# The second block's rows turned by VectorE, and the turn of x between the two low parts, in a fused attention and expert kernel

## The reference

```python
# attention: state = gamma * state + k v^T ; y = scale * q state
# layer 2:   h = relu(x @ w_in); x = (h * sigmoid(conv(h))) @ w_out
def _moe2_ref(x, w_gate, w_local, w1, w2):
    ...
            fresh_e = int(np.argmax(logits[b, s]))
            if s == 0 or local_gate[b, s] < 0.5:
                e = fresh_e
            else:
                e = prev_e if prev_e >= 0 else fresh_e
            ...
            h = np.maximum(x[b, s] @ w1[e], 0.0)
            out[b, s] = p[e] * (h @ w2[e])
```

## Time and profile before

| | us |
|---|---|
| median of 3 runs | 425.1 |
| lowest and highest run | 423.46, 425.39 |
| the profiled execution | 423.02 |
| its span, first to last instruction | 420.5 |
| TensorE busy in the span | 406.0 |
| VectorE busy | 238.8 |
| ScalarE busy | 211.0 |
| GpSimd busy | 100.7 |

### The profile page before, as it was taken

How to read it: one execution, slowest core, us unless ns; L and a number is a source line. 1 busy time by engine, 2 the same in 40 slices (tenths; PEclk the granted TensorE clock), 3 DMA queues, 4 the chain that set the end, 5 groups by cost and what they waited for, 6 DMA issues and landing times.

```text
span 420.5 us, 7363 instructions
## 1 busy us (share of the span) xinstructions
PE 406.0 (97%) x2637; PEld 333.1 (79%) x2638; DVE 238.8 (57%) x309; ACT 211.0 (50%) x293; POOL 100.7 (24%) x104
## 2 busy tenths in 40 slices
PE   7999999999999999999999999999989999999992
PEld 3888799887889987778787778787667878777782
DVE  4888749982004977686277622118773274663761
ACT  2344678670115764561557432338763284755661
POOL 3354782000000000027621412221122222031220
PEclk9999999999999999999999999999999999999998
DMA  8999900000520009555474932225786367493720
GB/s 292 408 410 416 383 1 2 0 2 0 200 101 0 2 0 389 211 202 163 130 287 149 400 129 94 75 100 203 299 311 244 100 235 307 128 399 127 258 87 4
DMA packets 28442, 76.16 MB, mean 181 GB/s; under 512 B 4927, under 2 KB 14399, under 8 KB 24064
## 3 DMA queue, kind: packets, MB, share of 16 engines
q1 hardware_dynamic: 25216, 67.26, 42.1%
q0 software_dynamic: 2912, 8.13, 5.8%
q10 hardware_dynamic: 288, 0.41, 0.3%
HBM read 62.68 MB, written 14.42 MB: 183 GB/s over the span
## 4 chain that ended last, share of the span: by engine, by line
PE 84%; ACT 7%; issue 3%; ACTq 1%; DMA 1%; DVE 1%; POOL 0%; DVEq 0%; POOLq 0%
PE ps L1039 23%; PE ps L1043 22%; PE ps L1040 22%; ACT wx L616 4%; PE ps L1312 4%; PE ps L1071 3%; PE ps L1092 3%; PE ps L1089 2%; PE ps L1055 1%; PE ps L1138 1%; DMA kv<-qkv 1%; ACT os L681 1%; DVE xF L957 1%; ACT hs L664 1%; ACT hT L674 1%
## 5 line engine op out<-in xcount | busy, mean ns | idle before, releaser
L970 DVE TENSOR_TENSOR hT<-ps,hT 128x512 fp32r<-128x512 f32 x34 | 23.5, 692 | 83.5 <-ACT hT L674 83.5
L951 DVE TENSOR_TENSOR wx<-raw_w,wx 128x1024 fp32r<-128x1024 f32 x56 | 65.1, 1220 | 2.8 <-ACT wx L616 2.8
L1039 PE MATMUL ps<-wx,hT 128*128 128x512 f32 x136 | 55.7, 409 | 0.3
L616 ACT CAST wx<-raw_w 128x1024 fp32r<-128x1024 f32 x56 | 55.0, 1046 | 0.0
L1043 PE MATMUL ps<-wx,hT 128*128 128x512 f32 x136 | 54.8, 403 | 0.0
L1043 PE MATMUL ps<-wx,xT 128*128 128x512 f32 x136 | 54.5, 401 | 0.0
L1039 PE MATMUL ps<-wx,xT 128*128 128x512 f32 x136 | 53.5, 393 | 0.0
L1040 PE MATMUL ps<-wx,hT 128*128 128x512 f32 x136 | 53.3, 392 | 0.0
L1040 PE MATMUL ps<-wx,xT 128*128 128x512 f32 x136 | 53.2, 391 | 0.0
L494 POOL DMA_INDIRECT out<-os,snow x16 | 18.8, 1176 | 104.9 <-ACT os L681 104.9
L1039 PE MATMUL ps<-x,win 128*128 128x384 f32 x128 | 43.2, 337 | 0.0
(11 more groups left out here) (165 smaller groups left out, 726.4 us busy)
## 6 DMA issues: line engine op xcount, KB each, us to landing
raw_w<-w_exp SPq DMA_DIRECT2D x28, 1024.0 KB, 7.1
qk<-qkv SPq DMA_DIRECT2D x7, 768.0 KB, 9.5
raw_first<-w_exp SPq DMA_DIRECT2D x4, 1024.0 KB, 7.7
x_block<-xg SPq DMA_DIRECT2D x16, 256.0 KB, 2.0
xq<-x_block SPq DMA_DIRECT2D x64, 64.0 KB
kv<-qkv SPq DMA_DIRECT2D x4, 768.0 KB, 11.2
x_rows<-x2n SPq DMA_DIRECT2D x11, 256.0 KB, 2.8
kv<-qkv SPq DMA_DIRECT2D x7, 384.0 KB, 10.0
```

Source lines behind the costliest of these rows:

```text
L616: nc.scalar.copy(wx[:, slot, 0, c], raw).then_inc(wx_hi[w], 1)
L951: nc.vector.tensor_tensor(wx[:, slot, 1, c], raw, wx[:, slot, 0, c].bitcast(F32), ALU.subtract).then_inc(w2_lo_dve if w else w1_lo_dve, 1)
L970: nc.vector.tensor_tensor(lo, psHT[:, 512 * a:512 * a + 512], hi.bitcast(F32), ALU.subtract).then_inc(hT_done, 1)
L1039: mm(o, lh, rl, start=first, stop=False)
```

## The change

- Block 1's rows are no longer turned by TensorE. SP's `step(0)` stores `xg` once both are there, `gathered` 32 and `x_first` 2 (the last x2 tile, over whose place `xq` lies, has been read by TensorE), and loads the quarters; VectorE turns them and ScalarE and VectorE take the high and low parts from `xF`, after both halves of block 0's h.
- SP issues both halves of `raw_w2` of expert 1 ahead of the last x2 half store, and `raw_w1` of expert 2 behind `step(0)`.
- VectorE's `turn_x(g+1)` goes between `h_lo(g,0)` and `h_lo(g,1)` in every block from 1 on.
- In an expert's first block ScalarE does relu(g,0) ahead of the evacuation, and h_hi(g,0) ahead of the last weight piece.
- In TensorE's first layer of block 0 the parts come in another order: the last rows go one part sooner, and the first half is complete after five parts instead of six.

```diff
@@ SP
                 if n == 0:
                     sp.wait_ge(gathered, 16)
-                    raw(1, 1, raw_w2, raw_w2_in, (0,))
+                    raw(1, 1, raw_w2, raw_w2_in)
             sp.wait_ge(x2_done, TT + 1)
-            sp.wait_ge(gathered, 32)
-            raw(1, 1, raw_w2, raw_w2_in, (1,))
-            raw(0, 2, raw_w1[0], raw_w1_in[0])
...
             def step(g):
                 sp.wait_ge(gathered, 16 * g + 32)
                 sp.wait_ge(x_turned, 16 * g + 32)
                 sp.dma_start(x_block, xg[:]).then_inc(x_stored, 16)
-                sp.wait_ge(x_stored, 16 * g)
+                sp.wait_ge(x_stored, 16 * g + 16)
                 for q in range(NQ):
                     sp.dma_start(xq[TR * q:TR * q + TR],
                                  x_block[:, P * q:P * q + P].rearrange("(b j) n -> j b n", j=TR)
                                  ).then_inc(quartered, 16)
+
+            sp.wait_ge(x_first, 2)
+            step(0)
+            raw(0, 2, raw_w1[0], raw_w1_in[0])
@@ GpSimd
-                pool.wait_ge(x_stored, 16 * g)
+                pool.wait_ge(x_stored, 16 * g + 16)
                 gather(g + 2)
...
             pool.wait_ge(tables, 1)
-            pool.wait_ge(gathered, 32)
-            pool.wait_ge(xg_free, 3)
+            pool.wait_ge(x_stored, 16)
             gather(2)
@@ ScalarE
             def first_step(g, e, slot):
+                relu(g, 0)
                 evac_before(g, o_done)
-                relu(g, 0)
+                h_hi(g, 0)
                 if e is not None:
                     weights_hi(0, e, slot, (3,))
-                h_hi(g, 0)
                 relu(g, 1)
                 h_hi(g, 1)
                 act.wait_ge(x_turned, 16 * g + 48)
-                x_hi(g + 1, xF[:].rearrange("p k t -> p (k t)"))
+                x_hi()
...
             relu(0, 1)
-            act.wait_ge(xg_free, 3)
-            x_hi(1, psXT)
             h_hi(0, 1)
+            act.wait_ge(x_turned, 48)
+            x_hi()
             weights_hi(0, 1, 1, (2, 3))
@@ VectorE
-            dve.sem_inc(x_turned, 48)
+            dve.sem_inc(x_turned, 32)
...
             def step(g):
                 h_lo(g, 0)
+                turn_x(g + 1)
                 h_lo(g, 1)
-                turn_x(g + 1, 64 * g)
-                x_lo(g + 1, xF[:].rearrange("p k t -> p (k t)"))
+                x_lo(g + 1)
...
             def first_step(g, e, slot):
                 h_lo(g, 0)
+                turn_x(g + 1)
                 if e is not None:
                     weights_lo(0, e, slot, (3,))
                 h_lo(g, 1)
-                turn_x(g + 1, 64 * g)
-                x_lo(g + 1, xF[:].rearrange("p k t -> p (k t)"))
+                x_lo(g + 1)
...
             h_lo(0, 0)
-            x_lo(1, psXT)
             h_lo(0, 1)
+            turn_x(1)
+            x_lo(1)
             weights_lo(0, 1, 1, range(4))
@@ TensorE
-                for k, a in ((0, 0), (0, 1), (1, 0), (1, 1), (2, 0), (3, 0), (2, 1), (3, 1)):
-                    if (k, a) == (1, 0):
+                for k, a in ((0, 0), (0, 1), (1, 0), (2, 0), (3, 0), (1, 1), (2, 1), (3, 1)):
+                    if (k, a) == (0, 1):
                         last_rows(TT - 1, TT + 1, (2, 3))
...
-                    if (k, a) == (2, 1):
+                    if (k, a) == (1, 1):
                         turn_h(0, 0)
...
             first_w1()
-            turn_x(gathered, 32)
             pe.wait_ge(o_done, 1)
```

More of the change, by code:

```diff
@@ L304, in build @@
         psEnd, psRow, psSlot, psInv = bank(6), bank(3), bank(7), bank(2)
-        psP1, psHT, psXT, psO = bank(0, 2), bank(2, 2), bank(4), bank(5)
+        psP1, psHT, psO = bank(0, 2), bank(2, 2), bank(5)
         def column_half(a, n):
@@ L386, in _, with step @@
                     sp.wait_ge(gathered, 16)
-                    raw(1, 1, raw_w2, raw_w2_in, (0,))
+                    raw(1, 1, raw_w2, raw_w2_in)
             sp.wait_ge(x2_done, TT + 1)
-            sp.wait_ge(gathered, 32)
-            raw(1, 1, raw_w2, raw_w2_in, (1,))
+            def step(g):
+                sp.wait_ge(gathered, 16 * g + 32)
+                sp.wait_ge(x_turned, 16 * g + 32)
+                sp.dma_start(x_block, xg[:]).then_inc(x_stored, 16)
+                sp.wait_ge(x_stored, 16 * g + 16)
+                for q in range(NQ):
+                    sp.dma_start(xq[TR * q:TR * q + TR],
+                                 x_block[:, P * q:P * q + P].rearrange("(b j) n -> j b n", j=TR)
+                                 ).then_inc(quartered, 16)
+            sp.wait_ge(x_first, 2)
+            step(0)
             raw(0, 2, raw_w1[0], raw_w1_in[0])
@@ L665, in relu, with x_hi @@
                                      ACT.Relu).then_inc(h_done, 1)
-            def x_hi(g, source):
-                nc.scalar.copy(xT[:, 0].rearrange("p k t -> p (k t)"), source).then_inc(xT_hi, 1)
+            def x_hi():
+                nc.scalar.copy(xT[:, 0].rearrange("p k t -> p (k t)"), xF[:].rearrange("p k t -> p (k t)")).then_inc(xT_hi, 1)
             def h_hi(g, a):
@@ L952, in weights_lo, with turn_x, x_lo @@
                                             ALU.subtract).then_inc(w2_lo_dve if w else w1_lo_dve, 1)
-            def turn_x(g, waited):
-                dve.wait_ge(quartered, waited)
+            def turn_x(g):
+                dve.wait_ge(quartered, 64 * g)
                 nc.vector.transpose(xF[:].rearrange("p k (q t) -> p k q t", q=NQ),
                                     xq[:].rearrange("p q (k i) -> p k q i", k=KD)).then_inc(x_turned, 16)
-            def x_lo(g, source):
+            def x_lo(g):
                 dve.wait_ge(xT_hi, g + 1)
-                nc.vector.tensor_tensor(xT[:, 1].rearrange("p k t -> p (k t)"), source,
+                nc.vector.tensor_tensor(xT[:, 1].rearrange("p k t -> p (k t)"), xF[:].rearrange("p k t -> p (k t)"),
                                         xT[:, 0].rearrange("p k t -> p (k t)").bitcast(F32),
@@ L1280, in _ @@
                                 inverse()
[L1281 to L1287, removed]
             def first_w1():
```

## The result

| | before | after |
|---|---|---|
| median, us (10 runs each) | 424.51 | 428.77 |
| lowest and highest run | 423.46, 425.39 | 426.02, 429.38 |
| ratio of the runs, 95% interval | | 1.0093 (1.0074 to 1.0112) |
| the profiled execution | 423.02 | 429.05 |
| its span | 420.5 | 426.7 |

The change costs 0.9%, 4.3 us, clear of the spread of the runs. The two profiles are 6.2 us apart: before's profiled execution lies 1.5 us under its median, after's 0.3 us over its own. What follows compares the profiles, so its terms add up to 6.2.

The account below looks back on a forecast made before the run. TensorE, with 84% of the chain, was taken as the bound. Terms +2.0, +0.3, +0.5, -2.1 and +0.2 sum to +0.9 us: 423.9 from the profiled 423.02, or 426.0 in the runs' terms; range 422.0 to 429.3.

Parts of the forecast that it names:

- Block 1: Blocks 1 to 3: rows by store, quarters and VectorE delay block 1's second layer 3.2 us, making block 3 2.0 late.
- the one term for the last x2 store: SP's queue before block 1's gather: store delayed 1.3 us behind raw_w2's second half, bounds 0 and 2.6.
- the 1.2 us of waits that was to come back: Blocks 1 to 3: existing waits of 1.2 us would vanish, since ScalarE is no longer behind there.
- Block 3's quarters: Block 3: quarter loads land late for the turn ahead of the second low part, +0.3 us, bounds 0 and +1.
- Blocks 7 to 9: Around experts 2 and 3: of 3.6 us to win nothing is kept, as block 9 waits for quarters; +0.5 us.
- the 12.7 of the text: Block 7 to block 8: time between turn starts falls to 12.7 us, 2.3 better than 14.97.
- this chain: Block 9 on SP: store, raw weights, store, quarters, then turn; it could come forward by 1.2 us, turn at 323.0.
- The changes behind: Three later expert changes: 0.7 us won each, -2.1 us, less +0.2 for late quarters at blocks 12 and 14.
- (5): Sign expected in the changed profile: block 9 to 16 takes 84 to 85 us instead of 86.
- C: Slower rival: quarters land late behind every expert change, in blocks 3, 9, 12 and 14; 429 us, chance 0.22.
- A: The forecast itself: gains and losses cancel; 426.0 us, own range 424.0 to 427.5, chance 0.45.
- D: Slower rival: raw_w2 halves delay the last x2 store 2.6 us, block 1 costs 3.3; 427.3 to 428 us, chance 0.11.

Follow-up runs that it names:

- the order alone: Kernel before with only ScalarE's new sequence in an expert's first block (relu ahead of evacuation, h_hi ahead of last weight piece): 424.83 us, ratio 1.0019.
- the last kernel: Kernel before with ScalarE's new sequence, gather ahead of scatter, and VectorE's turn between low parts in experts' first blocks only: 421.78 us, ratio 0.9933.
- the half loads: Changed kernel and kernel before, each with half of every raw weight load of experts 2 to 7 left out: 422.90 and 422.86 us.
- the turn alone: Kernel before with only VectorE's turn moved between the two low parts: 424.60 us, ratio 1.0002.
- the kernel with the path and the order: Changed kernel with VectorE's turn put back behind both low parts of h: 427.55 us, ratio 1.0087.
- the kernel with filled wait and low parts first: Changed kernel with turn behind low parts, 10 filling matmuls, and expert 1's two casts and three low parts ahead of block 1's turn: 427.39 us, 1.0079.
- the order with the gather first: Kernel before with ScalarE's new sequence and GpSimd's gather of block g+2 ahead of the scatter of block g-1: 421.26 us, ratio 0.9928.

## Why the forecast came out as it did

426.0 us was forecast, 0.9 us over before, with the likeliest case (0.46) at no measurable change. 428.77 us is inside the range, on the slower side, which had 0.32; but the change costs 4.3 us, not 0.9, and the range of 7.3 us held it by its width, not by the sum. By the steps:

**Block 1, right in mechanism, low by 1.5 us.** The store cost 2.0 us from SP, as taken from the rows. The estimate of 2.6 us went by a figure that the Trainium skill, "DMA: Bandwidth & Descriptors", "Anatomy of one DMA", gives for DMAs issued from GpSimd. Rows, turn and first layer came 0.6 to 0.7 us after their forecasts (208.4, 213.8, 216.1), all of it from the one term for the last x2 store: 2.0 us behind the second half of the raw load, where I had 1.3. What was late next was, as forecast, VectorE's low parts; the start of the second layer (223.75, forecast 223.0) follows. That is 0.7 us of the 1.5. The other 0.8 lies behind it: of the 1.2 us of waits that was to come back, only 0.35 did (from the start of the second layer to T(3) it takes 22.81 us instead of 23.16). The working had left out the turn of block 2's rows: its quarters came at 226.3 instead of 223.5, since the store stood in SP's queue behind 2 MB of raw weights for 7.1 us. The half clock was missing too, but there it is hidden.

**Block 3's quarters, +0.8 for +0.3.** The wait of 0.60 us ahead of part 4 is the one described; its size hung on a landing that I had only bounded.

**Blocks 7 to 9, the step that failed.** Up to block 8 the working held: T(7) to T(8) is 12.37 us for the 12.7 of the text (whose terms add up to 12.6). Block 9 waits where it was said to. But "this chain can come forward only as far as the weights' issue does: by 1.2 us" was wrong in its sign: the turn came 33.1 us after T(7), where it had come 32.8 us after it. Measured, the raw weights' issue came forward by 0.7 us against T(7), not 1.2, and the store behind them took 5.6 us instead of 3.7. The rows of SP show why a sooner issue behind the raw weights would not help: in all twelve kernels with whole loads this store lands 14.6 to 15.8 us after the raw weights' issue, though it is itself issued 6.8 to 11.7 us after them (before 317.03 for 306.19 and 320.76; changed 319.62, 309.62, 325.19; the order alone 317.73, 307.24, 322.91; the last kernel 313.07, 306.27, 321.08). That is what a store does that lands when SP's queue has run dry: in the kernel before the DMA engines are busy for 0.96 of the time from 318 to 320.7 us and for 0.30 of it from there to 323. The Trainium skill has this in "DMA: Bandwidth & Descriptors", "Queues, rings and completion order": SP's copies share one ring on each DMA engine, and descriptors are taken from it in ring order. The traces agree, and the half loads show it from the other side (2.0 us). Why it is 14.6 us in the kernel before and 15.6 us in the changed one stays open: scatter and gather fall into both stretches, and nearly the same bytes move in them (5.16 and 5.18 MB), at 354 and 333 GB/s.

**Half clock, not in the forecast at all:** 1.6 us behind block 9's wait, which there is on the path. It is the larger half of the 2.7 us that the term was short of; the wait itself, 3.9 us for some 3, is the rest with block 9's later rows.

**The changes behind, -1.4 for -1.9.** Kernels with the turn or the order or both have 72.4 to 72.7 us there against 74.06: 0.5 us in each change instead of 0.7. What the signs in the text called (5), 84 to 85 us from block 9 to 16, was a slip of its own, since block 9's wait lies inside (90.4 measured).

**The rivals.** C had the condition that decided in block 9, that the chain does not come forward with T, and I gave it half the chance of A. That its price of 429 us is the time measured is luck: it was made of 1 us each in blocks 3, 12 and 14 and 0.8 us more in block 9. In blocks 12 and 14 VectorE's turn waited 1.47 and 2.11 us and TensorE not at all, block 3 had 0.6 us, and the stretch with block 9 in it cost 2.7 us more than forecast. The delay of the gather, 1.3 us in the forecast and 2.6 us in D, was 2.0 us. What the text did not see is that the parts don't add up. Alone, neither the turn nor the order changes the time; together they cost 0.8%. The path on top adds 0.1%, though it costs some 2.5 us up to block 4 in the profiles; it was only ever added to the other two. The text took the gain of both parts at the changes of experts as one sum, so it couldn't see that either part alone has it. And it priced the turn's waits in blocks 1 and 3 at 0.3 us, where together they are 1.1 us in the changed kernel and 2.5 to 2.6 us with block 1's rows on TensorE.

## What to carry to other kernels

A gain that ends in a wait for a transfer is worth nothing, and the second such gain, or a wait that was put on an engine with no slack, is worth less than nothing if the clock falls behind it; so ask for every wait that is removed which transfer is next, and how far its landing stands from that point. In SP's queue here, the landing of a small store behind bulk loads was set by the issue of the bulk (14.6 to 15.8 us after it), not by its own. A load on which a small chain depends goes out ahead of the bulk, even at the price of a scatter that nobody waits for.

## What the runs showed of the hardware

After waits of 2.41 us (block 1) and 3.88 us (block 9) TensorE ran at a granted clock of 0.5 for about 3 us. The length of the wait by itself doesn't decide, and the 2.4 us that the expectation for the turn alone took as a border is none. It fell after the 2.03 us of block 8 in the kernel with the path and the order, but not after 2.29 us in the kernel before, nor after the 2.93 us of block 10 in the kernel with filled wait and low parts first. A window behind the first and one behind the last, in this order:

```profile
311.00:314.00 3.00, 3.00 (x12) 2.38 (x11) 1.13 (x1) 0.60 (x1) 2.17 (x3) 0.61 0.86 256
```

```profile
331.00:334.00 3.00, 2.81 (x12) 2.36 (x13) 0.00 (x0) 0.00 (x0) 1.45 (x3) 1.00 0.49 164
```

In one and the same execution, that of the turn alone, it fell to 0.51 behind 2.50 us (block 1) and stayed at 1.00 behind 2.48 us (block 9). Runs of one kernel differ too: the four of the order with the gather first had mean clocks of 0.997, 0.997, 0.991 and 0.991 and took 420.59, 420.66, 421.87 and 422.04 us; those of the kernel before range from 0.990 to 0.997, and its profile is one of 0.997. So a part of what two profiles differ by can be this, and not the edit. What decides it, these runs don't settle. Ten matmuls on zeros in the wait of block 1 kept the clock at 1.00.
